# Gated attention and two feed-forward layers on one core: out products of narrow steps two steps behind, and a reordered prologue

## The reference

```
for t in range(S):                       # gated linear attention, per batch and head
    m_new = max(f[t] + m, i[t])
    C = exp(f[t] + m - m_new) * C + exp(i[t] - m_new) * outer(v[t], k[t])
    n = exp(f[t] + m - m_new) * n + exp(i[t] - m_new) * k[t]
    y[t] = sigmoid(o[t]) * (C @ q[t]) / max(abs(n . q[t]), 1)
x  = y / sqrt(mean(y * y) + 1e-6) * rms_g            # 1536 x 320
x2 = (silu(x @ w_gate) * (x @ w_val)) @ w_out        # inner width 1536
out = leaky_relu(x2 @ w_in, 0.01) @ w_out2           # inner width 2048
```

## Time and profile before

| | us |
|---|---|
| median of 3 runs | 456.73 (455.63 to 456.83) |
| the profiled execution | 456.91 |
| its span, first to last instruction | 455.10 |
| PE busy in the span | 429.4 (94%) |
| DVE, ACT, POOL busy | 237.7, 195.6, 90.8 |
| first gate product starts | 28.67 |
| first wide gate product starts | 119.70 |

### The profile page before, as it was taken

How to read it: one execution, slowest core, us unless ns; L and a number is a source line. 1 busy time by engine, 2 the same in 40 slices (tenths; PEclk the granted TensorE clock), 3 DMA queues, 4 the chain that set the end, 5 groups by cost and what they waited for, 6 DMA issues and landing times.

```text
span 455.1 us, 8152 instructions
## 1 busy us (share of the span) xinstructions
PE 429.4 (94%) x3202; PEld 377.0 (83%) x3202; DVE 237.7 (52%) x439; ACT 195.6 (43%) x431; POOL 90.8 (20%) x92
## 2 busy tenths in 40 slices
PE   2769889999999999999999999999999999999997
PEld 1658878999978888888888888899999999999996
DVE  7556676667656565654743335534334334443534
ACT  1774663565526353423533224554343343333332
POOL 1455656412211111100333201441000000000000
PEclk9999989999999999999999999999999999999999
DMA  5876356331321250000122200310000000010101
GB/s 154 296 234 191 121 180 202 121 120 61 92 91 37 83 169 3 0 1 0 65 63 65 63 1 1 99 61 0 1 0 1 0 2 0 1 58 1 58 1 58
DMA packets 21444, 31.37 MB, mean 69 GB/s; under 512 B 1328, under 2 KB 15296, under 8 KB 21408
## 3 DMA queue, kind: packets, MB, share of 16 engines
q1 hardware_dynamic: 21408, 30.87, 21.4%
HBM read 28.85 MB, written 2.02 MB: 68 GB/s over the span
## 4 chain that ended last, share of the span: by engine, by line
PE 79%; issue 6%; POOL 5%; DMA 4%; DVE 2%; ACT 2%; SPq 1%; POOLq 0%; DVEq 0%; ACTq 0%
PE gate_ps L968 22%; PE value_ps L968 21%; PE out_ps L1040 9%; PE out_ps L1004 9%; PE turn_ps L1040 6%; POOL w_sb L397 3%; PE out_ps L1008 3%; PE c_ps L1040 3%; PE turn_ps L943 2%; DMA att_sb<-in_tok 1%; PE turn_ps L904 1%; DMA att_sb<-in_qk 1%; PE turn_ps L921 1%; POOL w_sb L399 1%; DMA decay_scratch<-acum 1%
## 5 line engine op out<-in xcount | busy, mean ns | idle before, releaser
L531 ACT ACTIVATE h_hi<-hid 128x512 fp32r<-128x512 f32 (+1 forms) x94 | 55.1, 586 | 115.0 <-DVE hid L767 76.3
L780 DVE TENSOR_TENSOR h_lo<-hid,h_hi 128x512 fp32r<-128x512 f32 (+1 forms) x94 | 69.8, 743 | 57.2 <-ACT h_hi L531 56.9
L968 PE MATMUL gate_ps<-x_hi,w_sb 128*128 128x512 f32 (+1 forms) x280 | 69.5, 371 | 4.5 <-DVE act_buf L761 3.5
L968 PE MATMUL value_ps<-x_hi,w_sb 128*128 128x512 f32 (+1 forms) x280 | 69.6, 371 | 0.0
L968 PEld LDWEIGHTS gate_ps<-x_hi,w_sb 128*128 128x128 f32 x280 | 47.7, 192 | 13.6 <-issue 4.4
L968 PEld LDWEIGHTS value_ps<-x_hi,w_sb 128*128 128x128 f32 x280 | 47.7, 193 | 6.2
L761 DVE SCALAR_TENSOR_TENSOR act_buf<-act_buf,gate_ps 128x512 f32<-128x512 f32 (+1 forms) x46 | 26.1, 568 | 47.4 <-ACT act_buf L519 47.4
L1004 PE MATMUL out_ps<-h_hi,w_sb 128*128 128x512 f32 (+1 forms) x184 | 47.6, 345 | 1.1 <-DVE h_lo L780 1.1
L519 ACT ACTIVATE act_buf<-gate_ps 128x512 f32<-128x512 f32 (+1 forms) x46 | 23.0, 499 | 47.3 <-PE gate_ps L968 47.2
L405 POOL TENSOR_TENSOR w_sb<-raw,w_sb 128x704 fp32r<-128x704 f32 x16 | 27.5, 1720 | 78.1 <-ACT w_sb L513 78.1
L1040 PE MATMUL out_ps<-w_sb,h_hi 128*128 128x320 f32 x192 | 42.9, 308 | 0.0
(11 more groups left out here) (138 smaller groups left out, 724.1 us busy)
## 6 DMA issues: line engine op xcount, KB each, us to landing
raw<-in_w SPq DMA_DIRECT2D x12, 544.0 KB, 5.3
expo<-decay_scratch SPq DMA_DIRECT2D x12, 512.0 KB, 5.5
att_sb<-in_tok SPq DMA_DIRECT2D x12, 484.0 KB, 5.4
raw<-in_w SPq DMA_DIRECT2D x16, 352.0 KB, 2.8
att_sb<-in_qk SPq DMA_DIRECT2D x24, 160.0 KB
out_y<-y_acc SPq DMA_DIRECT2D x12, 160.0 KB, 1.9
consts_sb<-in_consts SPq DMA_DIRECT2D x1, 129.5 KB, 3.0
gates_sb<-in_gates SPq DMA_DIRECT2D x1, 96.0 KB, 2.4
```

The source lines that it names most:

```text
L531: nc.scalar.activation(h_hi[:, r, 0:n], hid[:, r, 0:n], ACT.Copy).then_inc(hi_done, 1)
L780: nc.vector.tensor_tensor(h_lo[:, r, 0:n], hid[:, r, 0:n], h_hi[:, r, 0:n].bitcast(F32), ALU.subtract).then_inc(h_done, 1)
L968: last = nc.tensor.matmul(ps[:, 0:n], lhs, rhs, start=(j == 0), stop=(j == len(xs) - 1))
```

## The change

The out products of the narrow steps run two steps behind (`outs`), so `h_hi` and `h_lo` keep four narrow results (`slot`, each buffer in two halves). R, O and T of tiles 2 to 5 move by up to two steps. On DVE, `finish` is cut in two: `denominator` stays in front of `gated`, the rest goes behind it; `update_state` goes in front of `low`. On ACT, `ogate` and `hi_weights` go from the beginning of a step to its end, and tiles 2 and 3 are normalised a step later. On POOL, the weight remainders go in front of `fade_state`, and `inverse_rms` behind one more of them.

In the prologue SP loads raw weight piece 0 in front of the exponents, and the table of exponents in DRAM is laid out so that each partition's copy is one run of 4 KB instead of 8 runs of 512 B. ACT rounds weight piece 0 in front of the exponents, POOL weighs the keys of tiles 0 and 1 and takes the remainder of weight piece 1, and `x_high` of tile 0 goes to DVE.

```diff
-BESIDE = {2: (0, 1, 2, 3), 3: (3, 4, 5, 6), 4: (7, 8, 9, 10), 5: (10, 11, 12, 14), 6: (14, 15, 16, 17),
+BESIDE = {2: (0, 1, 2, 4), 3: (3, 5, 6, 8), 4: (7, 9, 10, 11), 5: (10, 12, 13, 14), 6: (14, 15, 16, 17),
...
+        def kept(n, z=1):
+            return 2 * n + z + 1 if n < FIRST else n + FIRST + 1
+        def at_once(n):
+            return BESIDE[n][3] == BESIDE[n][2] + 1
...
+        def narrow(s):
+            return s < STEPS1 and STEPS[s][1] * P < CHUNK
...
+        def slot(s):
+            c0 = (s // RING % 2) * (CHUNK // 2) if narrow(s) else 0
+            return s % RING, slice(c0, c0 + width(s))
...
+        def read_first(s):
+            return s - 2 * RING if narrow(s) else s - RING
+        def outs(s):
+            if narrow(s):
+                return (s - RING,) if s >= RING else ()
+            return (s - RING, s - 1) if narrow(s - 1) else (s - 1,)
...
-                b, t = n % 2, n // 2
-                src = scratch[b:b + 1, :, t * P:(t + 1) * P].broadcast_to([P, H, P])
-                sp.dma_start(expo[:, n % EXPO, :].rearrange("p (h t) -> p h t", h=H), src)\
-                    .then_inc(expo_in[n % EXPO], 16)
+                src = rows[n:n + 1, :].broadcast_to([P, H * P])
+                sp.dma_start(expo[:, n % EXPO, :], src).then_inc(expo_in[n % EXPO], 16)
...
             load_att(0)
             sp.wait_ge(a_done, 1)
-            sp.dma_start(rows[:, 0:P], acum[:, 0:P]).then_inc(scratch_out, 16)
+            sp.dma_start(sums[:, 0:1, :], by_time[:, 0:1, :]).then_inc(scratch_out, 16)
+            load_raw(0, W1RAW, w1[0, :, :])
             sp.wait_ge(scratch_out, 16)
             load_decays(0)
             load_decays(1)
             load_att(1)
-            load_raw(0, W1RAW, w1[0, :, :])
+            sp.wait_ge(a_done, 3)
+            sp.dma_start(sums[:, 1:, :], by_time[:, 1:, :]).then_inc(scratch_out, 16)
             load_raw(1, W1RAW, w1[1, :, :])
-            sp.wait_ge(a_done, 3)
-            sp.dma_start(rows[:, P:S], acum[:, P:S]).then_inc(scratch_out, 16)
             load_raw(2, W1RAW, w1[2, :, :])
             sp.wait_ge(scratch_out, 32)
             load_decays(2)
...
             def weigh_keys(n):
-                pool.wait_ge(last_done, n - FIRST + 1)
+                pool.wait_ge(last_done, kept(n))
...
             exponents(1)
             lo_weights(0)
+            weigh_keys(0)
+            weigh_keys(1)
+            lo_weights(1)
             inverse_rms(0)
             inverse_rms(1)
             exponents(2)
             lo_weights(2)
+            lo_weights(3)
             weigh_keys(2)
-            lo_weights(3)
+            exponents(3)
+            lo_weights(4)
             fade_state(2)
-            lo_weights(4)
-            exponents(3)
+            lo_weights(5)
             inverse_rms(2)
-            lo_weights(5)
             weigh_keys(3)
             lo_weights(6)
-            fade_state(3)
             lo_weights(7)
             exponents(4)
+            lo_weights(8)
+            fade_state(3)
+            lo_weights(9)
             inverse_rms(3)
-            lo_weights(8)
             weigh_keys(4)
-            lo_weights(9)
-            fade_state(4)
             lo_weights(10)
             exponents(5)
+            lo_weights(11)
+            fade_state(4)
             inverse_rms(4)
-            lo_weights(11)
             weigh_keys(5)
             fade_state(5)
             exponents(6)
...
+            def high1(s):
+                act.wait_ge(hid_done, after(s))
+                if read_first(s) >= 0:
+                    act.wait_ge(out_done, after(read_first(s)))
+                r, cols = slot(s)
+                nc.scalar.activation(h_hi[:, r, cols], hid[:, r, 0:width(s)], ACT.Copy).then_inc(hi_done, 1)
...
             ogate(0)
+            hi_weights(0)
             for n in range(FIRST):
                 for z in range(2):
                     decay(n, z)
+                    keep_last(n, slice(z, H, 2))
             ogate(1)
-            hi_weights(0)
+            hi_weights(1)
...
-            hi_weights(1)
+            hi_weights(2)
             square(0)
+            square(1)
             normalise(0)
-            square(1)
-            x_high(0)
             normalise(1)
             x_high(1)
-            for i in range(2, EARLY_W):
-                hi_weights(i)
+            first1(0, width(0))
+            hi_weights(3)
             for z in range(2):
                 decay(2, z)
             keep_last(2)
-            first1(0, width(0))
-            high(0, 0, width(0))
+            high1(0)
             for s in range(1, STEPS1 + 1):
                 work = beside(s - 1)
-                for n in work["R"]:
-                    ogate(n)
-                if EARLY_W + s - 1 < NF1:
-                    hi_weights(EARLY_W + s - 1)
                 if LAST1[-2] < s - 1 <= LAST1[-2] + GF:
...
+                for n in beside(s - 2)["O"] if s >= 2 else ():
+                    if not at_once(n):
+                        normalise(n)
                 for n in beside(s)["S"]:
                     decay(n, 1)
                     keep_last(n)
...
...
-                high(s, s % RING, width(s))
+                high1(s) if s < STEPS1 else high2(s, s % RING)
                 for n in work["O"]:
-                    normalise(n)
+                    if at_once(n):
+                        normalise(n)
                 for n in beside(s + 1)["S"]:
                     decay(n, 0)
+                for n in work["R"]:
+                    ogate(n)
+                if EARLY_W + s - 1 < NF1:
+                    hi_weights(EARLY_W + s - 1)
...
                                                   stab[:, c0 - 1:c0] if c0 else NEG, ALU.add, ALU.max))
+                if c0:
+                    first_table()
...
-            def lo_first(i):
...
-                if n < FIRST:
-                    dve.wait_ge(kw_done, n + 2 if n or z else 1)
-                else:
-                    dve.wait_ge(last_done, n - FIRST + 1)
+                dve.wait_ge(last_done, kept(n, z))
                 part = expo[:, n % EXPO, :].rearrange("p (q z t) -> p q z t", q=PAIRS, z=2)[:, :, z, :]
                 qk_ps = scores_ps(n, z)[:, :].rearrange("p (q t) -> p q t", q=PAIRS)
                 nc.vector.tensor_tensor(part, part, qk_ps, ALU.mult).then_inc(p_done, 1)
...
+            def first_x_high():
+                dve.wait_ge(consts_in, 16)
+                dve.wait_ge(t_done, 1)
+                for k in range(2):
+                    nc.vector.tensor_scalar(x_hi[:, k, 0:P], turned_ps(0)[:, k * P:(k + 1) * P], rms_sb[:, k:k + 1],
+                                            None, ALU.mult)
+                nc.vector.tensor_scalar(x_odd[0:ODD, 0:P], turned_ps(0)[0:ODD, 2 * P:3 * P], rms_sb[0:ODD, 2:3],
+                                        None, ALU.mult).then_inc(first_xhi, 1)
             def x_low(n):
-                dve.wait_ge(xhi_done, n + 1)
+                if n:
+                    dve.wait_ge(xhi_done, n)
+                else:
+                    dve.wait_ge(first_xhi, 1)
...
-            for z in range(2):
-                weigh_keys(0, slice(z, H, 2))
-                scores(0, z)
-            weigh_keys(1)
-            scores(1, 0)
-            scores(1, 1)
+            for n in range(FIRST):
+                for z in range(2):
+                    scores(n, z)
+            denominator(0)
             finish(0)
 
             dve.wait_ge(scratch_out, 32)
             dve.wait_ge(tab_ps, 2)
             nc.vector.memset(att_out(1)[0][:, DM:], ROOT_EPS)
+            denominator(1)
             finish(1)
             first_state(0)
-            lo_first(DVE_W)
+            first_state(1)
+            first_x_high()
             x_low(0)
-            first_state(1)
             x_low(1)
 
             gated(0, width(0))
             hidden1(0, width(0))
-            low(0, 0, width(0))
+            low1(0)
             for s in range(1, STEPS1 + 1):
                 work = beside(s - 1)
                 for n in work["S"]:
                     scores(n, 0)
                     scores(n, 1)
                 for n in work["O"]:
-                    finish(n)
+                    denominator(n)
                 if s < STEPS1:
                     gated(s, width(s))
+                for n in work["O"]:
+                    finish(n)
                 for n in work["R"]:
                     from_state(n)
                 if s < STEPS1:
                     hidden1(s, width(s))
                 else:
                     hidden2(s, s % RING)
+                for n in work["R"]:
+                    update_state(n)
                 for n in work["T"]:
                     x_low(n)
-                low(s, s % RING, width(s))
+                low1(s) if s < STEPS1 else low2(s, s % RING)
...
-                pe.wait_ge(kw_done, n + 2)
+                pe.wait_ge(kw_done, n + 1)
...
-            pe.wait_ge(xhi_done, FIRST)
```

(42 more changed lines are left out.)

51 lines of the change are left out of this document (19 added, 32 removed).

## The result

The changed kernel takes **453.50 us** (median of 10 runs, 451.60 to 455.19) against 456.05 (455.51 to 457.70, 10 runs). The ratio is 0.9943, with an interval of 0.9929 to 0.9956: 2.6 us faster. I had forecast 450.4, that is 6.3 faster. The time lies inside the wide range (446 to 455), outside the forecast's own range (448 to 452.5), and the gain is less than half of the forecast. The profiled execution took 455.19, with a span of 453.4.

A forecast was written before the change was run, and what follows sets the result against it. PE bounds the kernel from the first wide gate on; gains were open only in prologue and narrow phase. Prologue 2.0 off, narrow phase 5.2 off, clock 0.9 back: 6.3 off, 450.4 us; own range 448 to 452.5, 8-in-10 range 446 to 455.

The forecast's parts named there:

- rival C: Narrow phase: weights come too late, gates 4 to 12 take 9 us longer than forecast; 459 us, chance 0.06.
- The power: Prologue, POOL's power of one column: 0.55 us instead of 1.56, so 1.0 us off, bounds 0 to 1.0.
- rival B: Prologue: POOL is the bound, with more work in front of `inverse_rms`; 452 us, chance 0.08.
- The landing: Prologue: with 4 KB runs tile 1 lands 0 to 1.3 us earlier, taken as 1.0 us off.
- Raw weight piece 0: Prologue: its load in front of the exponents flows in a DMA hole, cost 0; up to 0.5 us back if it runs over.
- The out delay: Narrow phase: removes the 1.1 us wait for `h_lo` but takes a cover away; gates 0 to 5 lose 4.4 us, not 5.4.
- the clock: In front of gate(2): PE idles about 1.8 us and the clock may fall; 0.9 us back, ends 0 and 1.7.
- Gates 5 to 8: Narrow phase: POOL no longer held at `inverse_rms`, buffers free about one step earlier; 0.3 us lost instead of 4.2.
- Gates 8 to 20: End of the narrow phase: 2.4 us lost instead of 2.7.
- Tile 4's 1.4: Gates 8 to 20: wait for normalised tile 4, whose O moves to pass 10 behind scores(5) on DVE; taken as 1.4 us.
- Rival A: Narrow phase: the waits only move, 9 to 11 us of loss remain; 453.5 us, chance 0.18.
- D: Whole kernel: nothing comes of the change, gain and new waits cancel; 456.7 us, chance 0.04.

The follow-up runs named there:

- the version with the other two edits: Changed kernel with raw weight piece 0 loaded behind tile 1 and tile 5's scores one pass later, out products still two behind: 450.65 us, ratio 0.9861.

## Why the prediction was wrong, step by step

**What bounds the kernel: right.** Nothing moved behind the first wide gate, and all gain and loss lies in the 119.70 us before it. (By the kernel, the list has 46 steps, 20 to 45 wide, the second layer 48, and weight pieces 10 and 11 are first read at gates 20 and 21; the counts ahead of the prediction, 41, 96 and steps 0 to 11, are wrong. They enter no sum; rival C could press on gates 4 to 9 only.)

**The power, 1.0 off: right** (0.55). POOL stood idle for 1.09 in front of it, so it was not held by remainders either, and rival B is out.

**The landing, 1.0 off from the 4 KB runs: right in size** (0.7 to 1.1 alone, as read above). **Raw weight piece 0, "I take 0": this step failed first.** I had seen a hole from 7 to 8 and put 544 KB into it, at no cost, or 0.5 at most if it ran over. The DMA engines of the kernel before were in fact idle from 7 to 9 (columns as in rows 1):

```profile
7.00:9.00 2.00, 1.74 (x16) 1.44 (x14) 1.97 (x3) 0.47 (x1) 0.00 (x0) 1.00 0.01 4
```

Even so the piece got in the way. ACT got it at 9.13, and the exponents came 5.9 us after their issue, instead of 3.7 before and 4.4 with the piece behind. It cost 2.0 at gate(0) and about 1.5 in the time. So the prologue won 0.4 instead of 2.0: my sign of being wrong, gate(0) later than 28, came true. Why it costs 2 isn't shown: 544 KB at the 409 GB/s of the earlier trace rows would be 1.4 us, an estimate, and would have fitted.

**The out delay: this step failed second.** I had gates 0 to 5 at 4.4 lost instead of 5.4, and 0.9 back for the clock: about even. By itself the delay costs 2.2 us, and 1.7 in the version with the other two edits. The lost cover is one out product, 0.96, in front of gate(2); PE's idle time there goes from 0.40 to about 2 us in the traces that have the wait. The way from gate(0) to gate(3), less its floor (11.0 us one behind, 10.1 two behind, with one out product less), sorts the twelve traces that have the one order or the other throughout:

| gates 0 to 3, us lost | traces |
|---|---|
| one behind | 3.6, 3.7, 3.7, 4.8 |
| two behind, no fall of the clock behind gate(2) | 4.4, 4.7, 4.7, 4.8, 4.8 |
| two behind, with it | 7.0, 7.3, 7.5 |

The means are 4.0 and 5.7, so the delay costs about 1.7 us by these traces, an estimate, in line with the 2.2 and 1.7 measured. (I leave out the trace with only out(0) early and the one with the scores moved.) In the trace of the changed kernel 0.7 more than forecast is lost in front of gate(2) and 1.4 behind it. What decides whether the clock falls is open: it fell behind 1.94 to 2.11 us of idle time in three traces, and not behind 1.93 in another.

**Gates 5 to 8, 3.9 off: right in size (4.3), in part wrong in cause.** I gave it to POOL's `inverse_rms` and called ACT's new place nearly the same. Either reordering alone is enough, and both undone bring the loss back.

**Gates 8 to 20: 3.6 lost instead of 2.4.** Tile 4's 1.4 was right (1.5). Missed was the row `x_odd` L795: tile 3's turn moved from pass 7 to pass 9, and gate(10) is the first that reads its columns (0.7). The rest is 0.2 at each of the turns of tiles 5 and 6 and 0.1 here and there.

In the profiled execution the misses are 1.6 (prologue), 2.1 (gates 0 to 5), 1.2 (8 to 20), less 0.3 (5 to 8): 4.6, which is 455.19 - 450.6. Rival A (the waits only move, 453.5) named the time and part of what happened: 10.9 us were lost, inside its 9 to 11, and the wait for `gated` came back at gate(2) with the clock's fall. But the loss at gates 5 to 8 did not move, it went; 2.0 us more were lost at gates 0 to 5, by the delay that A held to touch little, and 0.9 more at 8 to 20, and A had nothing on the weight piece. C and D did not occur: no gate of the changed kernel waits for a remainder.

## What to carry to other kernels

Idle time of the DMA engines does not make a load free: a bulk load in front of critical ones on the same queue cost 2 us here although its bytes over the rate of the trace would have fitted. Try it in both places before it stays in front. An in-order queue stalls by what it waits for in front of urgent work, and two orders can each hide the same stall, so undo them together before one of them is called the cause. A product held back is a cover taken away: look first at which wait it stood in. And before a wait seen in one trace is called the effect of an edit, see whether the work in front of it ran at the same pace in both traces.

## What the runs showed of the hardware

- After an idle 2.07 us of PE the granted clock was 0.50, the 1.2 GHz level, from about 39 to 45 us, with PE busy all the time. With waits of 0.37 us at the same place it stayed at 1.00, and so it did after an idle 1.93 us in the kernel with the delay alone. The idle time before it doesn't decide it by itself.
- At gate(0) four matmuls of 256 columns take 1.19 to 1.22 us in all traces but one (1.00), and 0.64 later. The profile gives a granted clock of 1.00 for this in the kernel before and the changed one, and 0.50 for the same 1.19 in the run with piece 0 behind tile 1: the pace has to be read from the matmuls there. In five traces gate(1), about 6 us later, takes 1.22 as well.
- Two broadcast loads of 512 KB in runs of 512 B against 4 KB: what was queued behind them reached PE 6.8 to 6.9 us after its issue with the short runs, and 6.0 to 6.3 with the long ones. With 544 KB more in front on the same queue it was 7.9 to 8.7.
